# A three-stage fp32 chain on one core: two of four k-times-v products one step later, and a reordered change of stages

## The chip, the cores and the metric

The kernel runs on 1 core of one Trainium2 chip. The time is that of the device for one execution, in microseconds (us): 924.01 as the median of 3 runs (923.23 to 927.03). The engines have these names in the profile: PE is TensorE's matmuls and PEld its weight loads, DVE is VectorE, ACT is ScalarE, POOL is GpSimd, SP is the engine that issues the transfers (its queue reads SPq).

## The reference

```
kv  = einsum('bhsd,bhse->bhde', k, v)          # B=4, H=8, S=576, D=64
out = einsum('bhsd,bhde->bhse', q, kv)
rms = sqrt(mean(out * out, axis=-1) + 1e-6)
x   = out / rms * g_norm                       # then heads side by side: x is [2304, 512]
g   = x @ w_gate;  silu = g / (1 + exp(-g))    # w_gate, w_val: [512, 1536]
y   = (silu * (x @ w_val)) @ w_out             # w_out: [1536, 512]
h   = y @ w_in2                                # [512, 2048]
z   = (max(h, 0) + log1p(exp(-|h|))) @ w_out2  # [2048, 512]; the output, fp32
```

## The kernel before

There are three stages. The attention of batch 0 comes first (the first 35 us). Stage 1 is the gated layer: 6 chunks of 384 tokens (`NCH`) by 12 slices of 128 hidden columns (`NF1`), 72 steps k = 0..71, each with a chunk c and a slice f. The attention of batches 1 to 3 is laid between the steps of stage 1. Stage 2 is the second layer: 6 chunks by 16 slices (`NF2`).

Every matmul of the two layers is done in three passes on numbers split into a high part (rounded to the matmul's own format, fp32r) and a low part (the rest): lines L543, L544, L545. So each weight slice and each chunk of x has to be split first. For a weight slice, SP loads the raw numbers into one of two buffers (`stage1` or `stage2`), ACT copies them to the high part (L674 for stage 1, `split_high2` L681 for stage 2), and POOL subtracts that from the raw ones for the low part (L428, which counts `w_ready`). Only then may SP load the next slice but one into that buffer. The last slice of stage 2, f = 15, has both parts from POOL (L433 and L428). The slices of stage 2 take the places in `arena` that those of stage 1 leave: slice f may be written once the `down1` of a given step has been done (`slot_free2`).

A step k of stage 1 on PE is: gate(k), 12 matmuls into bank 0; val(k), 12 matmuls into bank 1; and down1(k-1), 12 matmuls that multiply the product of the step before by w_out. ACT makes silu of the gate (L695), DVE the gated product (`glu`: L881, then the split into g_hi at L872 and g_lo at L874). down1(k) waits for g_lo of step k (`g_split`).

Attention of batch b = 1, 2, 3: k times v of four pairs of heads (`pair`, L466, 20 small matmuls each). Pair 0 stands behind the gate of step `KV_AT[b]` (4, 17, 30), pair 1 behind its val, and pairs 2 and 3 both behind the gate of the next step. Pairs 0 and 2 share one buffer for k and v, pairs 1 and 3 another, so SP can issue the loads of pair 2 only when the product of pair 0 is done, and so for 3 and 1 (`next_pair`). DVE then copies the four products from PSUM into `kv_blocks` (`fill_blocks`, L773), two steps behind `KV_AT[b]` PE multiplies the first tile of q by it (`q_times_kv`, L481), and four more tiles follow, every second step. q comes turned by DVE (`turn_q`, L789).

SP works through one list in order. Around the attention of batch 1 that list is: weight slices 5, 6 and 7 of stage 1, then pairs 2 and 3 of batch 1, then slices 8 to 11.

At the change of stages (k = 71), before:

- PE: gate(71), val(71), down1(70), then up2(0,0) (stage 2, chunk 0, slice 0), then down1(71), then up2(0,1), up2(0,2), and from there up2 and down2 in turn. up2(0,0) needs the split x of chunk 0 (`xs_ready`), tile by tile, four tiles.
- DVE: the glu of step 70, then the split of x for stage 2 (`split_x`, L848 and L850 for each of four tiles), then the glu of step 71, then the softplus pieces of stage 2 (L892 to L899 and its own g_hi, g_lo). Tile t of the split may overwrite x_hi and x_lo once val(71) has read that tile (`xs_used`, `val_done`).
- ACT: silu(70), the high parts of slices 13 and 14, silu(71), the table of functions for stage 2, the four functions of the first softplus (L715 to L721), and then `store_y` (L705, four copies), which takes the sums of stage 1's last chunk out of PSUM.
- POOL: the low parts of slices 12, 13 and 14, and both parts of slice 15.

Of the kernel before, what the change touches and what calls it, by code (L numbers as in the profile page):

```python
# [45 lines left out]
BLK = 32  # L46
CB, BB = CH // BLK, S // BLK
POOL_HIGH = 1
ACT_HIGH2 = NF2 - 1
NATT = B - 1  # L50


# [25 lines left out]
def program(nc, ctx, q, k, v, g_norm, w_gate, w_val, w_out, w_in2, w_out2, out):  # L78
# [101 lines left out]
    def sem(name):  # L180
        return ctx.enter_context(nc.semaphore(name))
# [29 lines left out]
    w_hi_ready = sem("w_hi_ready")  # L211
    w_hi_ready_pool = sem("w_hi_ready_pool")
    w_ready = sem("w_ready")


    xs_hi_ready = sem("xs_hi_ready")
# [72 lines left out]
    def _(sp):  # L289
# [51 lines left out]
            sp.dma_start(stage1[:, s, 2 * KT * P:RAW1], w_out[f * P:(f + 1) * P, :]).then_inc(raw_loaded[s], 16)  # L341

        def load_step2(f):
            sp.wait_ge(w_ready, NF1 + f - 1)
            if f == 0:

                sp.wait_ge(kv_done, B * KT)
                sp.wait_ge(xn_ready, B * NT)
            s = f % 2
            sp.dma_start(stage2[:, s, 0:KT * P].rearrange("p (t n) -> p t n", t=KT),  # L350
                         w_in2[:, f * P:(f + 1) * P].rearrange("(t p) n -> p t n", p=P)).then_inc(raw_loaded[s], 16)
            sp.dma_start(stage2[:, s, KT * P:RAW2], w_out2[f * P:(f + 1) * P, :]).then_inc(raw_loaded[s], 16)
# [25 lines left out]
        load_q_blocks(1, 3)  # L378
        load_step1(5)
        load_step1(6)  # L380
        load_step1(7)
        next_pair(1, 2)
        next_pair(1, 3)
        for f in range(8, NF1):
            load_step1(f)
        for b in range(1, B):
            for j in range(3):
# [28 lines left out]
    @block.gpsimd  # L416
    def _(pool):
        nc.gpsimd.memset(eps[:, :], EPS).then_inc(zeros_ready, 1)
        nc.gpsimd.memset(kv_blocks[:, :, :], 0.0).then_inc(zeros_ready, 1)
        nc.gpsimd.memset(ident[:, :], 0.0).then_inc(zeros_ready, 1)  # L420
        pool.wait_ge(zeros_ready, 3)
        nc.gpsimd.affine_select(out=ident[:, :], in_=ident[:, :], compare_op=ALU.not_equal, fill=1.0, base=0,
                                pattern=[[-1, P]], channel_multiplier=1).then_inc(const_ready, 1)

        def split_rest(high, count, slot, raw, size):

            pool.wait_ge(high, count)
            nc.gpsimd.tensor_tensor(slot[:, size:2 * size], raw, slot[:, 0:size].bitcast(F32),  # L428
                                    ALU.subtract).then_inc(w_ready, 1)

        def split(n, count, slot, raw, size):
            pool.wait_ge(raw_loaded[n % 2], raw_count(n))
            nc.gpsimd.tensor_copy(slot[:, 0:size], raw).then_inc(w_hi_ready_pool, 1)  # L433
            split_rest(w_hi_ready_pool, count, slot, raw, size)

        for f in range(NF1):
            slot, raw = arena[:, f * SLOT1:(f + 1) * SLOT1], stage1[:, f % 2, :]
            if f < POOL_HIGH:  # L440
                split(f, f + 1, slot, raw, RAW1)
            else:
                split_rest(w_hi_ready, f - POOL_HIGH + 1, slot, raw, RAW1)
        for f in range(NF2):
            pool.wait_ge(down_done, slot_free2(f))
            slot, raw = arena[:, f * SLOT2:(f + 1) * SLOT2], stage2[:, f % 2, :]
            if f < ACT_HIGH2:
                split_rest(w_hi_ready, NF1 - POOL_HIGH + f + 1, slot, raw, RAW2)
            else:
                split(NF1 + f, POOL_HIGH + f - ACT_HIGH2 + 1, slot, raw, RAW2)  # L450


    @block.tensor
    def _(pe):
# [63 lines left out]
        def attention_after_gate(k):  # L518

            if k == 1:  # L520
                pe.wait_ge(x_ready, NT)
            for b in range(1, B):
                if k == KV_AT[b]:
                    pair(b, 0)
                if k == KV_AT[b] + 1:
                    pair(b, 2)
                    pair(b, 3)

# [60 lines left out]
        def up2(c, f):  # L589


            pe.wait_ge(w_ready, NF1 + f + 1)
            for t in range(KT):
                if f == 0:
                    pe.wait_ge(xs_ready, c * KT + (NCH * KT + t + 1))
# [26 lines left out]
        for k in range(1, STEPS1):  # L622
            up1(k)
            down1(k - 1)
        pe.wait_ge(silu_ready, STEPS1)
        up2(0, 0)
        down1(STEPS1 - 1)
        for f in range(1, LAG2):
            up2(0, f)
        with pe.Fori(0, NCH - 1) as c:  # L630
            for f in range(LAG2, NF2):
# [14 lines left out]
    def _(act):  # L646
# [92 lines left out]
        for k in range(1, STEPS1):  # L739
# [6 lines left out]
                root(b * NT, j)  # L746
            if k + 2 < NF1:
                split_high(k + 2)
            for f in range(ACT_HIGH2):
                if STEPS1 - NF1 + under(f) + 1 == k:  # L750
                    split_high2(f)
        nc.scalar.preload_act_table_set("natural_log_exp_and_others")
        softplus_terms(0, 0)
        store_y(NCH - 1)
        softplus_terms(0, 1)
        with act.Fori(0, NCH - 1) as c:
            for f in range(2, NF2):
# [10 lines left out]
    def _(dve):  # L768
# [107 lines left out]
        def glu(k):  # L876
# [6 lines left out]
            dve.wait_ge(g_ready, k + 1)  # L883
            split_g(k, 0, act_a[:, f % 2, :], g_hi[:, f % 2, :], g_lo[:, f % 2, :])

        def softplus(c, f):


# [16 lines left out]
        for k in range(STEPS1):  # L905
            c, f = divmod(k, NF1)
            for b in range(1, B):
                if k == KV_AT[b] + 1:
                    fill_blocks(b * KT, kv_ps)
            if k in TILE_OF:  # L910
                turn_q(*TILE_OF[k])
# [1 line left out]
                dve.wait_ge(x_ready, X_NEEDED[c + 1])  # L913
                split_x(c + 1, bass.ds(c * CB + CB, CB), val_done, k + 1)
            elif f == NF1 - 1:
                dve.wait_ge(acc_free, 2)
                split_x(NCH, bass.ds(0, CB), val_done, STEPS1, scaled=False)
            glu(k)
            if k in TILE_OF:
                b, j = TILE_OF[k]  # L920
# [1 line left out]
                normalize_turned(b, j)  # L922
            if k - TURN_AFTER in TILE_OF:
                turn_x(*TILE_OF[k - TURN_AFTER])
        with dve.Fori(0, NCH - 1) as c:
            for f in range(NF2 - 1):
                softplus(c, f)
# [27 lines left out]
```

## Time and profile before

| | |
|---|---|
| time, median of 3 runs | 924.01 us (923.23 to 927.03) |
| the profiled execution | 926.35 us, of which the span is 924.3 us and 2.05 us lie around it |
| PE busy in the span | 902.5 us (98%), 5128 matmuls |
| DVE busy | 526.9 us (57%) |
| ACT busy | 346.9 us (38%) |
| POOL busy | 84.6 us (9%) |
| mean granted clock of TensorE | 0.994 of full speed |
| chain that ended last | PE 91%, SPq 3%, DMA 2%, DVE 2%, POOL 1%, ACT 1% |

The busy time counts an instruction from its start to its end, and the matmuls overlap (one of 0.33 us starts every 0.17 us), so the start times on PE tell more than the busy share: where two rows of PE stand further apart than the matmuls between them take, PE stood still or ran slowly. The granted clock says at which share of 2.4 GHz TensorE ran in a stretch. The three stretches in which PE stands still for want of data, the start apart, lie at 64 to 70 us, at 161 us and at 511 to 519 us.

### The profile page before, as it was taken

How to read it: one execution, taken by the hardware profiler on the slowest of the kernel's cores; microseconds unless marked ns; L12 is line 12 of the kernel's file. 1: busy time of each engine (PE TensorE's matmuls, PEld its weight loads, DVE VectorE, ACT ScalarE, POOL GpSimd, SP SyncE). 2: the span in 40 equal slices, each digit the busy share in tenths (PEclk: the TensorE clock that was granted, in tenths of full speed). 3: DMA queues.
4: the chain of work that ended last, by engine and by line, in shares of the span. 5: the costliest groups of instructions: out<-in, count | busy, mean ns of one | idle time of the engine just before them, and what ended most of it. 6: DMA issues, size and time to landing. Idle time of an engine off the chain costs nothing.

```text
span 924.3 us, 13268 instructions
## 1 busy us (share of the span) xinstructions
PE 902.5 (98%) x5128; PEld 853.0 (92%) x5128; DVE 526.9 (57%) x1006; ACT 346.9 (38%) x602; POOL 84.6 (9%) x38
## 2 busy tenths in 40 slices
PE   6889999999999999999999899999999999999998
PEld 5779999999999999999999799998988998998997
DVE  3634652363245424214223887877878878878875
ACT  1433440243023301000233454545554544654543
POOL 2453300000000000000355200000000000000000
PEclk9999999999999999999999999999999999999999
DMA  9783362016211110000134000000000000000000
GB/s 222 171 198 92 93 137 64 23 35 143 59 23 46 39 42 1 1 1 1 45 116 137 23 1 1 34 0 0 34 0 0 34 0 0 34 0 0 35 1 35
DMA packets 84201, 44.38 MB, mean 48 GB/s; under 512 B 40768, under 2 KB 76736, under 8 KB 84160
## 3 DMA queue, kind: packets, MB, share of 16 engines
q1 hardware_dynamic: 84000, 43.80, 18.1%
q8 instruction: 30, 0.49, 0.2%
q14 instruction: 11, 0.09, 0.0%
q10 hardware_dynamic: 160, 0.00, 0.0%
HBM read 35.52 MB, written 8.26 MB: 47 GB/s over the span
## 4 chain that ended last, share of the span: by engine, by line
PE 91%; SPq 3%; DMA 2%; DVE 2%; POOL 1%; ACT 1%; issue 0%; DVEq 0%; ACTq 0%
PE bank L543 22%; PE bank L544 22%; PE bank L545 22%; PE bank L611 7%; PE bank L612 7%; PE bank L610 7%; PE bank L481 2%; SPq L316 1%; PE bank L466 1%; DMA v_rest<-in_v 1%; SPq L294 1%; POOL arena L428 1%; DVE x_lo L850 1%; SPq L339 1%; DMA v<-in_v 1%; DMA stage<-in_moe_w_out 0%
## 5 line engine op out<-in xcount | busy, mean ns | idle before, releaser
L543 PE MATMUL bank<-x_hi,arena 128*128 128x384 f32 x960 | 324.2, 338 | 5.6 <-DVE x_lo L850 3.5
L545 PE MATMUL bank<-x_hi,arena 128*128 128x384 f32 x960 | 322.7, 336 | 0.0
L544 PE MATMUL bank<-x_lo,arena 128*128 128x384 f32 x960 | 322.1, 336 | 0.0
L543 PEld LDWEIGHTS bank<-x_hi,arena 128*128 128x128 f32 x960 | 180.8, 188 | 12.5 <-DVE x_lo L850 3.7
L544 PEld LDWEIGHTS bank<-x_lo,arena 128*128 128x128 f32 x960 | 180.9, 188 | 3.8
L545 PEld LDWEIGHTS bank<-x_hi,arena 128*128 128x128 f32 x960 | 180.7, 188 | 0.0
L881 DVE TENSOR_TENSOR act_a<-act_a,bank 128x384 f32<-128x384 f32 x72 | 39.8, 553 | 231.5 <-PE bank L545 225.5
L695 ACT ACTIVATE act_a<-bank 128x384 f32<-128x384 f32 x72 | 35.3, 490 | 247.1 <-PE bank L545 246.8
L428 POOL TENSOR_TENSOR arena<-stage,arena 128x1024 fp32r<-128x1024 f32 (+1 forms) x28 | 80.8, 2895 | 414.0 <-ACT arena L681 370.1
L715 ACT ACTIVATE act_a<-bank 128x384 f32<-128x384 f32 x96 | 47.3, 493 | 189.1 <-PE bank L545 187.1
L612 PE MATMUL bank<-arena,g_lo 128*128 128x512 f32 x288 | 113.8, 395 | 0.0
L611 PE MATMUL bank<-arena,g_hi 128*128 128x512 f32 x288 | 113.6, 394 | 0.0
L610 PE MATMUL bank<-arena,g_hi 128*128 128x512 f32 x288 | 111.9, 389 | 0.0
L874 DVE TENSOR_TENSOR g_lo<-act_a,g_hi 128x384 fp32r<-128x384 f32 x168 | 100.2, 596 | 5.8
L543 PE MATMUL bank<-g_hi,arena 128*128 128x384 f32 x288 | 98.2, 341 | 0.0
L544 PE MATMUL bank<-g_lo,arena 128*128 128x384 f32 x288 | 96.4, 335 | 0.0
L545 PE MATMUL bank<-g_hi,arena 128*128 128x384 f32 x288 | 96.4, 335 | 0.0
L892 DVE SCALAR_TENSOR_TENSOR act_c<-act_w,act_u 128x384 f32<-128x384 f32 x96 | 53.4, 557 | 60.1 <-ACT act_w L719 60.1
L872 DVE CAST g_hi<-act_a 128x384 fp32r<-128x384 f32 x168 | 71.6, 426 | 7.6
L612 PEld LDWEIGHTS bank<-arena,g_lo 128*128 128x128 f32 x288 | 54.0, 187 | 11.5
L611 PEld LDWEIGHTS bank<-arena,g_hi 128*128 128x128 f32 x288 | 54.0, 188 | 9.3
L610 PEld LDWEIGHTS bank<-arena,g_hi 128*128 128x128 f32 x288 | 54.1, 188 | 8.8
(55 smaller groups left out, 795.6 us busy)
## 6 DMA issues: line engine op xcount, KB each, us to landing
stage<-in_moe_w_out SPq DMA_DIRECT2D x28, 256.0 KB, 3.4
out_dram<-out_stage SPq DMA_DIRECT2D x18, 256.0 KB, 2.1
k<-in_k SPq DMA_DIRECT2D x16, 256.0 KB, 3.2
v<-in_v SPq DMA_DIRECT2D x16, 256.0 KB, 3.3
stage<-in_moe_w_in SPq DMA_DIRECT2D x16, 256.0 KB, 2.6
xy<-in_q SPq DMA_DIRECT2D x48, 72.0 KB, 3.0
stage<-in_moe_w_gate SPq DMA_DIRECT2D x12, 256.0 KB, 3.3
stage<-in_moe_w_val SPq DMA_DIRECT2D x12, 256.0 KB, 3.5
```

The source lines that it names most:

```text
L428: nc.gpsimd.tensor_tensor(slot[:, size:2 * size], raw, slot[:, 0:size].bitcast(F32), ALU.subtract).then_inc(w_ready, 1)
L543: nc.tensor.matmul(ps, hi, rhs_hi, start=first, stop=False)
L544: nc.tensor.matmul(ps, hi, rhs_lo, start=False, stop=False)
L545: return nc.tensor.matmul(ps, lo, rhs_hi, start=False, stop=last)
L610: nc.tensor.matmul(acc_ps[t][:, :], g[0], w[0], start=(f == 0), stop=False)
L611: nc.tensor.matmul(acc_ps[t][:, :], g[0], w[1], start=False, stop=False)
L612: last = nc.tensor.matmul(acc_ps[t][:, :], g[1], w[0], start=False, stop=(f == NF2 - 1))
L715: nc.scalar.activation(a, hid_ps[f % RING2][:, 0:CH], ACT.Abs).then_inc(abs_ready, 1)
L872: nc.vector.tensor_copy(hi, g).then_inc(g_hi_ready, 1)
L874: nc.vector.tensor_tensor(lo, g, hi.bitcast(F32), ALU.subtract).then_inc(g_split, 1)
L881: nc.vector.tensor_tensor(act_a[:, f % 2, :], act_a[:, f % 2, :], val_ps[:, 0:CH], ALU.mult).then_inc(g_ready, 1)
L892: nc.vector.scalar_tensor_tensor(act_c[:, :], w, 1.0, u, ALU.subtract, ALU.subtract).then_inc(rest_ready, 1)
```

## The change

Attention: the products of pairs 2 and 3, and DVE's `fill_blocks` behind them, move from step `KV_AT[b] + 1` to `KV_AT[b] + 2` (steps 6, 19 and 32), the step in which the first q tile is multiplied. In SP's list the loads of pairs 2 and 3 of batch 1 come ahead of weight slice 7 and no longer behind it.

Change of stages: on PE down1(71) comes ahead of up2(0,0). On DVE the glu of step 71 comes ahead of the split of x. The low parts of slices 13, 14 and 15 are made by DVE (`split_late`, with a count of its own, `w_late_ready`) and no longer by POOL: 13 and 14 ahead of the glu of step 71, 15 behind the split of x. The high part of slice 15 is made by ACT as the others are, and `store_y` comes ahead of the first softplus.

DVE, the end of step 4 to the beginning of step 6 (act_a<-act_a,bank is the gated product, kv_blocks the copy of `fill_blocks`, q_t the turned q). Before:

```order
L881 TENSOR_TENSOR act_a<-act_a,bank 128x384
L872 CAST g_hi<-act_a 128x384
L874 TENSOR_TENSOR g_lo<-act_a,g_hi 128x384
L773 COPY kv_blocks<-bank 64x4x64 x2
L881 TENSOR_TENSOR act_a<-act_a,bank 128x384
L872 CAST g_hi<-act_a 128x384
L874 TENSOR_TENSOR g_lo<-act_a,g_hi 128x384
L789 STREAM_TRANSPOSE q_t<-xy 128x4x4x32
```

After:

```order
L884 TENSOR_TENSOR act_a<-act_a,bank 128x384
L875 CAST g_hi<-act_a 128x384
L877 TENSOR_TENSOR g_lo<-act_a,g_hi 128x384
L884 TENSOR_TENSOR act_a<-act_a,bank 128x384
L875 CAST g_hi<-act_a 128x384
L877 TENSOR_TENSOR g_lo<-act_a,g_hi 128x384
L776 COPY kv_blocks<-bank 64x4x64 x2
L792 STREAM_TRANSPOSE q_t<-xy 128x4x4x32
```

The copies to `kv_blocks` have moved behind the glu of step 5, right ahead of the first turn of q.

DVE at the change of stages, from the end of the glu of step 70 on (x_hi and x_lo are the split of x, arena<-stage_118,arena is a low part of a weight slice). Before:

```order
L874 TENSOR_TENSOR g_lo<-act_a,g_hi 128x384
L848 CAST x_hi<-xy 128x384
L850 TENSOR_TENSOR x_lo<-xy,x_hi 128x384
L848 CAST x_hi<-xy 128x384
L850 TENSOR_TENSOR x_lo<-xy,x_hi 128x384
L848 CAST x_hi<-xy 128x384
L850 TENSOR_TENSOR x_lo<-xy,x_hi 128x384
L848 CAST x_hi<-xy 128x384
L850 TENSOR_TENSOR x_lo<-xy,x_hi 128x384
L881 TENSOR_TENSOR act_a<-act_a,bank 128x384
L872 CAST g_hi<-act_a 128x384
L874 TENSOR_TENSOR g_lo<-act_a,g_hi 128x384
```

After:

```order
L877 TENSOR_TENSOR g_lo<-act_a,g_hi 128x384
L893 TENSOR_TENSOR arena<-stage_118,arena 128x1024 x2
L884 TENSOR_TENSOR act_a<-act_a,bank 128x384
L875 CAST g_hi<-act_a 128x384
L877 TENSOR_TENSOR g_lo<-act_a,g_hi 128x384
L851 CAST x_hi<-xy 128x384
L853 TENSOR_TENSOR x_lo<-xy,x_hi 128x384
```

Two low parts and the glu now stand ahead of the split of x, whose other three tiles follow, and behind them the third low part.

ACT at the same place, from the high parts of slices 13 and 14 on (act_a<-bank is first silu(71), then the first function of the softplus; xy<-bank is `store_y`). Before:

```order
L681 ACTIVATE arena<-stage_118 128x1024 x2
L695 ACTIVATE act_a<-bank 128x384
L752 ACT_TABLE_LOAD
L715 ACTIVATE act_a_0_97<-bank 128x384
L717 ACTIVATE act_u_0_98<-act_a_0_97 128x384
L719 ACTIVATE act_w_0_105<-act_u_0_98 128x384
L721 ACTIVATE act_a_0_97<-act_w_0_105 128x384
L705 ACTIVATE xy<-bank 128x12x32 x4
```

After:

```order
L684 ACTIVATE arena<-stage_118 128x1024 x2
L698 ACTIVATE act_a<-bank 128x384
L684 ACTIVATE arena<-stage_118 128x1024
L755 ACT_TABLE_LOAD
L708 ACTIVATE xy<-bank 128x12x32 x4
L718 ACTIVATE act_a_0_97<-bank 128x384
L720 ACTIVATE act_u_0_98<-act_a_0_97 128x384
L722 ACTIVATE act_w_0_105<-act_u_0_98 128x384
```

The high part of slice 15 and the four copies of `store_y` now stand ahead of the first softplus.

```diff
--- before.py
+++ after.py
@@ -46,7 +46,8 @@
 BLK = 32
 CB, BB = CH // BLK, S // BLK
 POOL_HIGH = 1
-ACT_HIGH2 = NF2 - 1
+
+LATE2 = NF2 - 3
 NATT = B - 1
 
 
@@ -211,6 +212,7 @@
     w_hi_ready = sem("w_hi_ready")
     w_hi_ready_pool = sem("w_hi_ready_pool")
     w_ready = sem("w_ready")
+    w_late_ready = sem("w_late_ready")
 
 
     xs_hi_ready = sem("xs_hi_ready")
@@ -341,7 +343,10 @@
             sp.dma_start(stage1[:, s, 2 * KT * P:RAW1], w_out[f * P:(f + 1) * P, :]).then_inc(raw_loaded[s], 16)
 
         def load_step2(f):
-            sp.wait_ge(w_ready, NF1 + f - 1)
+            if f - 2 >= LATE2:
+                sp.wait_ge(w_late_ready, f - 1 - LATE2)
+            else:
+                sp.wait_ge(w_ready, NF1 + f - 1)
             if f == 0:
 
                 sp.wait_ge(kv_done, B * KT)
@@ -378,10 +383,9 @@
         load_q_blocks(1, 3)
         load_step1(5)
         load_step1(6)
-        load_step1(7)
         next_pair(1, 2)
         next_pair(1, 3)
-        for f in range(8, NF1):
+        for f in range(7, NF1):
             load_step1(f)
         for b in range(1, B):
             for j in range(3):
@@ -441,13 +445,10 @@
                 split(f, f + 1, slot, raw, RAW1)
             else:
                 split_rest(w_hi_ready, f - POOL_HIGH + 1, slot, raw, RAW1)
-        for f in range(NF2):
+        for f in range(LATE2):
             pool.wait_ge(down_done, slot_free2(f))
             slot, raw = arena[:, f * SLOT2:(f + 1) * SLOT2], stage2[:, f % 2, :]
-            if f < ACT_HIGH2:
-                split_rest(w_hi_ready, NF1 - POOL_HIGH + f + 1, slot, raw, RAW2)
-            else:
-                split(NF1 + f, POOL_HIGH + f - ACT_HIGH2 + 1, slot, raw, RAW2)
+            split_rest(w_hi_ready, NF1 - POOL_HIGH + f + 1, slot, raw, RAW2)
 
 
     @block.tensor
@@ -522,7 +523,7 @@
             for b in range(1, B):
                 if k == KV_AT[b]:
                     pair(b, 0)
-                if k == KV_AT[b] + 1:
+                if k == KV_AT[b] + 2:
                     pair(b, 2)
                     pair(b, 3)
 
@@ -589,7 +590,10 @@
         def up2(c, f):
 
 
-            pe.wait_ge(w_ready, NF1 + f + 1)
+            if f >= LATE2:
+                pe.wait_ge(w_late_ready, f + 1 - LATE2)
+            else:
+                pe.wait_ge(w_ready, NF1 + f + 1)
             for t in range(KT):
                 if f == 0:
                     pe.wait_ge(xs_ready, c * KT + (NCH * KT + t + 1))
@@ -622,10 +626,9 @@
         for k in range(1, STEPS1):
             up1(k)
             down1(k - 1)
+        down1(STEPS1 - 1)
         pe.wait_ge(silu_ready, STEPS1)
-        up2(0, 0)
-        down1(STEPS1 - 1)
-        for f in range(1, LAG2):
+        for f in range(LAG2):
             up2(0, f)
         with pe.Fori(0, NCH - 1) as c:
             for f in range(LAG2, NF2):
@@ -746,12 +749,12 @@
                 root(b * NT, j)
             if k + 2 < NF1:
                 split_high(k + 2)
-            for f in range(ACT_HIGH2):
+            for f in range(NF2):
                 if STEPS1 - NF1 + under(f) + 1 == k:
                     split_high2(f)
         nc.scalar.preload_act_table_set("natural_log_exp_and_others")
+        store_y(NCH - 1)
         softplus_terms(0, 0)
-        store_y(NCH - 1)
         softplus_terms(0, 1)
         with act.Fori(0, NCH - 1) as c:
             for f in range(2, NF2):
@@ -883,6 +886,13 @@
             dve.wait_ge(g_ready, k + 1)
             split_g(k, 0, act_a[:, f % 2, :], g_hi[:, f % 2, :], g_lo[:, f % 2, :])
 
+        def split_late(f):
+
+            slot = arena[:, f * SLOT2:(f + 1) * SLOT2]
+            dve.wait_ge(w_hi_ready, NF1 - POOL_HIGH + f + 1)
+            nc.vector.tensor_tensor(slot[:, RAW2:SLOT2], stage2[:, f % 2, :], slot[:, 0:RAW2].bitcast(F32),
+                                    ALU.subtract).then_inc(w_late_ready, 1)
+
         def softplus(c, f):
 
 
@@ -905,7 +915,7 @@
         for k in range(STEPS1):
             c, f = divmod(k, NF1)
             for b in range(1, B):
-                if k == KV_AT[b] + 1:
+                if k == KV_AT[b] + 2:
                     fill_blocks(b * KT, kv_ps)
             if k in TILE_OF:
                 turn_q(*TILE_OF[k])
@@ -913,8 +923,8 @@
                 dve.wait_ge(x_ready, X_NEEDED[c + 1])
                 split_x(c + 1, bass.ds(c * CB + CB, CB), val_done, k + 1)
             elif f == NF1 - 1:
-                dve.wait_ge(acc_free, 2)
-                split_x(NCH, bass.ds(0, CB), val_done, STEPS1, scaled=False)
+                split_late(LATE2)
+                split_late(LATE2 + 1)
             glu(k)
             if k in TILE_OF:
                 b, j = TILE_OF[k]
@@ -922,6 +932,9 @@
                 normalize_turned(b, j)
             if k - TURN_AFTER in TILE_OF:
                 turn_x(*TILE_OF[k - TURN_AFTER])
+        dve.wait_ge(acc_free, 2)
+        split_x(NCH, bass.ds(0, CB), val_done, STEPS1, scaled=False)
+        split_late(LATE2 + 2)
         with dve.Fori(0, NCH - 1) as c:
             for f in range(NF2 - 1):
                 softplus(c, f)
```

## Rows read from the trace of the kernel before

**Rows 1.** Waits of PE: engine line, waited for: us in total, times, longest
```profile
PE bank L466 <- DMA v_rest<-in_v: 11.2, 4, 6.7
```

**Rows 2.** Timeline of PE, 63 to 82 us: start, length, instruction, [idle before it, releaser]
```profile
63.73 0.34 PE L545 MATMUL bank<-x_hi,arena 128*128 128x384 f32 x1
67.25 1.12 PE L466 MATMUL bank<-v,k 128*64 128x64 f32 x16 [3.18 <-DMA v_rest<-in_v]
...
70.65 0.69 PE L543 MATMUL bank<-x_hi,arena 128*128 128x384 f32 x1
...
73.85 0.33 PE L543 MATMUL bank<-g_hi,arena 128*128 128x384 f32 x1
...
80.09 1.05 PE L481 MATMUL bank<-kv_blocks,q_t 128*128 128x128 f32 x8
```

**Rows 3.** Timeline of PE, 158 to 167 us
```profile
159.72 0.34 PE L545 MATMUL bank<-x_hi,arena 128*128 128x384 f32 x1
...
162.74 0.44 PE L543 MATMUL bank<-x_hi,arena 128*128 128x384 f32 x1
```

**Rows 4.** Timeline of PE, 249 to 256 us
```profile
250.77 0.34 PE L545 MATMUL bank<-x_hi,arena 128*128 128x384 f32 x1
...
252.79 0.44 PE L543 MATMUL bank<-x_hi,arena 128*128 128x384 f32 x1
```

**Rows 5.** Timeline of SP, 60 to 68 us
```profile
61.53 0.43 SPq L294 DMA_DIRECT2D k<-in_k  x1
...
65.85 0.61 SPq L297 DMA_DIRECT2D v_rest<-in_v  x1
```

**Rows 6.** Timeline of POOL, 66 to 71 us
```profile
67.09 3.43 POOL L428 TENSOR_TENSOR arena<-stage,arena 128x1536 fp32r<-128x1536 f32 x1 [3.52 <-ACT arena L674]
```

**Rows 7.** Timeline of DVE, 160 to 168 us
```profile
162.86 0.88 DVE L773 COPY kv_blocks<-bank 64x256 f32<-64x256 f32 x2 [6.39 <-PE bank L466]
...
166.66 0.70 DVE L789 STREAM_TRANSPOSE q_t<-xy 128x512 f32<-128x512 f32 x1
```

**Rows 8.** Timeline of PE, 507 to 523 us
```profile
511.31 0.34 PE L545 MATMUL bank<-g_hi,arena 128*128 128x384 f32 x1
...
516.69 0.69 PE L543 MATMUL bank<-x_hi,arena 128*128 128x384 f32 x1 [3.00 <-DVE x_lo L850]
...
521.63 0.33 PE L543 MATMUL bank<-x_hi,arena 128*128 128x384 f32 x1
```

**Rows 9.** Busy time by stretch (us, PE PEld DVE ACT POOL, PEclk, DMA share, GB/s)
```profile
516.00:520.00 4.00, 3.28 (x9) 2.73 (x10) 2.85 (x6) 0.95 (x2) 0.22 (x1) 0.57 0.02 4
```

**Rows 10.** Timeline of DVE, 503 to 525 us
```profile
503.43 0.55 DVE L881 TENSOR_TENSOR act_a<-act_a,bank 128x384 f32<-128x384 f32 x1 [3.65 <-PE bank L545]
...
504.41 0.56 DVE L874 TENSOR_TENSOR g_lo<-act_a,g_hi 128x384 fp32r<-128x384 f32 x1
...
509.31 2.66 DVE L850 TENSOR_TENSOR x_lo<-xy,x_hi 128x384 fp32r<-128x384 f32 x1
...
512.28 0.56 DVE L850 TENSOR_TENSOR x_lo<-xy,x_hi 128x384 fp32r<-128x384 f32 x1
...
523.54 0.56 DVE L874 TENSOR_TENSOR g_lo<-act_a,g_hi 128x384 fp32r<-128x384 f32 x1
```

**Rows 11.** Timeline of POOL, 500 to 517 us
```profile
501.24 2.43 POOL L428 TENSOR_TENSOR arena<-stage,arena 128x1024 fp32r<-128x1024 f32 x1 [2.27 <-ACT arena L681]
506.64 4.92 POOL L428 TENSOR_TENSOR arena<-stage,arena 128x1024 fp32r<-128x1024 f32 x2 [2.98 <-ACT arena L681]
...
513.82 2.41 POOL L428 TENSOR_TENSOR arena<-stage,arena 128x1024 fp32r<-128x1024 f32 x1
```

**Rows 12.** Timeline of ACT, 505 to 523 us
```profile
507.12 1.07 ACT L681 ACTIVATE arena<-stage 128x1024 fp32r<-128x1024 f32 x1 [0.62 <-DMA stage<-in_moe_w_out]
...
508.57 1.28 ACT L752 ACT_TABLE_LOAD   x1
519.02 0.49 ACT L715 ACTIVATE act_a<-bank 128x384 f32<-128x384 f32 x1 [9.16 <-PE bank L545]
```

## The prediction

> **What bounds the kernel now.** The page comes first: PE is busy for 98% of the span and the chain that ended last is 91% PE. So only what makes PE stand still, or run slowly, is worth time. The table of PE's waits names the transfer of k and v as the largest [rows 1]: 11.2 us in four waits, of which the longest, 6.7 us, belong to the loads at the very start, which the change leaves alone. The timeline of PE then shows where it loses time, and I measure that between starts, since a matmul's length overlaps the next. Undisturbed, 36 matmuls take 80.09 - 73.85 = 6.24 us, so one takes 0.1733 us [rows 2].
>
> Three places stand out. At 64 us PE waits for k and v of pairs 2 and 3 of batch 1 [rows 2], at 161 us for those of batch 2 [rows 3], at 511 us for the split x of stage 2 [rows 8]. Batch 3 passes the same place with no wait [rows 4]. Behind a stand of 3.00 us [rows 8] the granted clock is low: from 516 to 520 us it is 0.57 on the mean, so mostly the lower level of 1.2 GHz [rows 9].
>
> **Batch 1.** The gate of step 5 ends at 63.73 + 0.17 = 63.90, and down1(4) begins at 73.85 [rows 2]. Between them lie two products (40 small matmuls) and val(5): 9.95 us. Undisturbed, the two products cost 252.79 - 250.94 = 1.85 us (batch 3, [rows 4]), val 12 x 0.1733 = 2.08, and the first matmul behind them starts its successor about 0.1 late (0.44 long in place of 0.33). That is 4.03. The loss is 5.9 us: the waits, and val at the lower clock (from 70.65 to 73.85 its 12 matmuls took 3.20 and not 2.08).
>
> After the change PE runs val(5), down1(4) and gate(6), 36 matmuls, before it wants pairs 2 and 3: at 63.90 + 6.24 = 70.14, with its usual gap at 70.4. In the trace both pairs had landed about a microsecond before PE went on at 70.65 [rows 2], although their eight issues, from 61.53 to 65.85 + 0.61 = 66.46 [rows 5], stood behind the three of weight slice 7. SP now issues them ahead of those, so they land 1.5 us earlier at least. The wait goes whole: gain 5.9, lower bound 5.
>
> What the move pushes back is slice 7. At worst its three issues end where the pairs' ended, 66.46 in place of 61.5, 5 us later. Its low part was ready at 67.09 + 3.43 = 70.52 [rows 6], so then at 75.5. up1(7) begins after the products (1.95), val(6), the q tile (0.8) and down1(5), at about 77.1. Slice 7 is hidden, by 1.6 us in the worst case.
>
> DVE's copies to kv_blocks (0.88) now stand straight ahead of the turn of q (0.70) [rows 7], and both must be through before the first q tile. They start 0.12 behind the products and last 1.58, so they end 1.70 behind; PE has val in between, 2.08 and 0.1. Margin 0.5 us, at steps 6, 19 and 32. Behind the waiting copies DVE has the turn and the glu of the same step, which needs val anyway. Cost 0; from below nothing can be gained there, from above it is the margin overrun, taken up as a rival.
>
> **Batch 2.** 162.74 - 159.89 = 2.85 us for two products [rows 3] against 1.85. SP's issues stay where they are and PE comes a step, 6.24 us, later. Gain 1.0. **Batch 3** had no wait: 0.
>
> **Change of stages.** down1(70) ends at 511.48, up2(0,1) begins at 521.63 [rows 8]. Between them lie the 24 matmuls of up2(0,0) and down1(71), 4.16 us undisturbed; it took 10.15. The loss is 5.99, the most this part can give. I follow DVE to see what stays.
>
> Two x_lo of the same shape take 0.56 and 2.66 us [rows 10]; the long one ran from 509.31 to 511.97, while POOL was in its low parts, 506.64 to 511.56, and a second one as long beside POOL's of 513.82 [rows 11]. After the change POOL's last work is slice 12, over at 501.24 + 2.43 = 503.67. So DVE works at its short times. The Trainium skill (SBUF — State Buffer, "SBUF: two separate sides") says why: VectorE and GpSimd share one port pair as an exclusive lock, taken by a VectorE operation with two SBUF inputs against a GpSimd one that reads SBUF. By that rule moving three low parts from POOL to DVE takes the blocking away for the whole change of stages; were it a slowness of DVE's own there, the sum would be that of the second rival. The rows agree with the rule so far.
>
> A low part on DVE (1024 elements) is in no row. Bounds: 0.56 (384 elements, [rows 10]) and POOL's 2.43 [rows 11]. ACT's copies of these sizes stand as 1.07 to 0.49 [rows 12]; 0.56 x 1.07 / 0.49 = 1.22, in proportion to the elements it would be 1.49. I take 1.22. The Trainium skill (VectorE: DVE Perf Modes, "The TRN2 errata") gives (N + 151) / 0.96 ns for such a subtraction, an estimate of 1.22 as well; no row here shows it.
>
> Slice 13 can start when POOL started it, 506.64, slice 14 when ACT's copy ends, 507.12 + 1.07 = 508.19 [rows 11, 12]. DVE is through with both at 508.25 + 1.22 = 509.5. The glu of step 71 follows that of step 70 by 6.24: 503.43 + 6.24 = 509.67 [rows 10], when val(71) is done. So they fit, by 0.2. g_lo ends 504.97 - 503.43 = 1.54 later, at 511.21, and PE wants it at 511.48: no stall, margin 0.27.
>
> Then the split of x: cast and subtraction are at most 1.54 - 0.55 = 0.99 a tile, so the tiles are ready at 512.2, 513.2, 514.2, 515.2. PE, with down1(71) ahead, wants them at 513.56, 514.08, 514.60, 515.12. Only the last is close, 0 to 0.1 us.
>
> Next in line is the first softplus. SP may load slice 15 when DVE has slice 13 done, 507.9; before, it was at 509.1, and POOL had cast it and gone on at 513.82, about 3.6 us after issue plus a cast of 1.1. So it lands at 511.5. ACT may write its place when down1(70) is done, 511.65; copy 1.07, table 1.28, four copies of `store_y` at most 0.49 each [rows 12]: ACT is free at 516.0 at the latest. up2(0,0) ends at 515.64, so ACT costs 0.1. From the first function to g_lo took 524.10 - 519.02 = 5.08 [rows 10, 12]: 521.1. PE wants it after three more up2, at 515.64 + 6.24 = 521.88. Margin 0.8. The third low part fits in DVE's wait before it. Where the stall goes, nothing else is late.
>
> **Sum.** 5.9 + 1.0 + 6.0 = 12.9; 0.2 off for the two tight handovers: 12.7. Span 924.3 - 12.7 = 911.6, with the 2.05 around it 913.65 for the profiled execution. That execution (926.35) was 2.3 above the median of the runs, 924.01, so against the median the forecast is **911.3**.
>
> **Rivals.**
> (A) A low part on DVE takes its upper bound, 2.43. Then both are done at 506.64 + 4.86 = 511.5, g_lo at 513.0, PE stands 1.5 us, the tiles of x follow at PE's pace. 912.8. For it: no row of the operation. Against: ACT's ratio.
> (B) The long x_lo is not POOL's doing. Then the split begins at 511.2 and goes as slowly as before: the third tile came 516.69 - 509.31 = 7.4 us after the first x_lo began, so at about 519, wanted at 514.6; 4.4 lost and 1 more at the lower clock. 916.7. Against: 0.56 at 512.28, in POOL's pause between 511.56 and its cast.
> (C) The 5.9 of batch 1 is given back at the weights: PE reaches up1(7) to up1(11) 6 us earlier, and the two raw buffers, ACT and POOL may not keep up. 917.2. Against: in ACT's order slice 8 and later stand behind the functions of PE's own q tiles, so they move with PE; slice 7 is hidden by 1.6.
> (D) Slower. At steps 6, 19 and 32 PE waits for kv_blocks and the turned q, with down1 queued behind. It decides from 0.5 us of lateness on DVE, one to one, three times. To eat 12.7 us DVE must be 4.7 late at each; at 5.5 late it is 15 lost, 926.3. Against: DVE is idle for 6.39 us ahead of its copies [rows 7], and POOL, which could stretch DVE, works only near the first of the three.
> (E) The change does not do what it says, both waits stay: 924.
>
> **How the numbers follow.** Forecast 0.77, A 0.10, B 0.04, C 0.06, D 0.01, E 0.02. A change under 0.5% (4.6 us) could not be told from none. Faster: forecast, A, B, C and some of D's small cases, 0.97; same 0.02; slower 0.01. The range, 909.7 to 916.0, takes the whole 12.9, 1.4 for the spread of such medians (the runs before lie 923.23 to 927.03), and A with as much above it, most of what B and C lose.
>
> **What the profile after would show.** Right: no wait for k and v but at the start; two products in step 6, at about 70.4 us; val at 0.1733 a matmul; the L853 subtractions at 0.56 throughout; a low part on DVE of about 1.2 us, two of them over by 502.6 (509.5 less 6.9); no PEclk below 1.00 after the start. Wrong: PE rows with a wait for `w_ready` in steps 7 to 11, for kv_blocks or q_t in steps 6, 19, 32, for g_lo at the change, or x_lo still over 2 us with POOL at rest.

## The result, and the profile after

The changed kernel takes 913.30 us in the median of 4 runs (912.77 to 915.10), the kernel before 925.26 in 4 runs beside it (923.23 to 927.03). The ratio is 0.9869, 95% interval 0.9848 to 0.989: 1.3% faster. The profiled execution took 912.80 us with a span of 911.0 and a mean granted clock of 1.00 (before: 926.35, 924.3 and 0.994).

The page of the changed kernel, PE's row of part 1 and the chain that ended last:

```profile
PE 896.5 (98%) x5128; PEld 849.2 (93%) x5128; DVE 524.8 (58%) x1009; ACT 348.1 (38%) x603; POOL 76.0 (8%) x34
...
PE 97%; DVE 1%; SPq 1%; DMA 1%; ACT 0%; issue 0%; ACTq 0%
```

PE's busy time is 6.0 us less: 2.3 of it lie in the stretch of batch 1 and 2.5 at the change of stages, where matmuls ran at the lower clock or were drawn out by a wait, and 0.8 lie in the first 38 us, which the change leaves alone. The chain is now 97% PE. PE's two longest waits in the span (answers to [rows 1]):

```profile
PE bank L467 <- DMA v_rest<-in_v: 6.9, 1, 6.9
PE bank L544 <- DVE x_lo L848: 1.9, 3, 0.9
```

The 11.2 us in four waits for v_rest have become one of 6.9, the loads at the very start. L848 is the split of x for stage 1, in the first steps; L853, that for stage 2, is no longer among them.

Step 6 of the changed kernel on PE (answers to [rows 2]): the last matmul of gate(6), the two products, val(6), the first q tile.

```profile
69.57 0.34 PE L546 MATMUL bank<-x_hi,arena 128*128 128x384 f32 x1
69.84 0.69 PE L467 MATMUL bank<-v,k 128*64 128x64 f32 x16
...
70.71 0.69 PE L467 MATMUL bank<-v,k 128*64 128x64 f32 x16
...
71.59 0.44 PE L544 MATMUL bank<-x_hi,arena 128*128 128x384 f32 x1
...
73.78 0.94 PE L482 MATMUL bank<-kv_blocks,q_t 128*128 128x128 f32 x7
```

From 69.57 + 0.17 to 71.59 are 1.85 us, the undisturbed price of [rows 4]. DVE beside it (answers to [rows 7]):

```profile
71.71 0.88 DVE L776 COPY kv_blocks<-bank 64x256 f32<-64x256 f32 x2 [4.32 <-PE bank L467]
72.62 0.71 DVE L792 STREAM_TRANSPOSE q_t<-xy 128x512 f32<-128x512 f32 x1
74.48 0.55 DVE L884 TENSOR_TENSOR act_a<-act_a,bank 128x384 f32<-128x384 f32 x1 [1.15 <-PE bank L546]
```

The copies start 0.12 behind the products and the turned q is ready at 73.33; PE wants it at 73.78. Margin 0.45.

The change of stages, PE: last matmul of down1(70), first of down1(71), last of it, first of up2(0,0) and of up2(0,1) (answers to [rows 8]).

```profile
503.98 0.33 PE L546 MATMUL bank<-g_hi,arena 128*128 128x384 f32 x1
504.15 0.33 PE L544 MATMUL bank<-g_hi,arena 128*128 128x384 f32 x1
...
506.06 0.33 PE L546 MATMUL bank<-g_hi,arena 128*128 128x384 f32 x1
506.23 0.33 PE L544 MATMUL bank<-x_hi,arena 128*128 128x384 f32 x1
...
508.31 0.33 PE L544 MATMUL bank<-x_hi,arena 128*128 128x384 f32 x1
```

24 matmuls in 508.31 - 504.15 = 4.16 us; it was 10.15. DVE there (answers to [rows 10]):

```profile
499.20 1.23 DVE L893 TENSOR_TENSOR arena<-stage,arena 128x1024 fp32r<-128x1024 f32 x1 [1.56 <-ACT arena L684]
500.97 1.22 DVE L893 TENSOR_TENSOR arena<-stage,arena 128x1024 fp32r<-128x1024 f32 x1 [0.55 <-ACT arena L684]
502.34 0.55 DVE L884 TENSOR_TENSOR act_a<-act_a,bank 128x384 f32<-128x384 f32 x1
...
503.32 0.56 DVE L877 TENSOR_TENSOR g_lo<-act_a,g_hi 128x384 fp32r<-128x384 f32 x1
...
506.78 0.56 DVE L853 TENSOR_TENSOR x_lo<-xy,x_hi 128x384 fp32r<-128x384 f32 x1
...
513.04 0.56 DVE L877 TENSOR_TENSOR g_lo<-act_a,g_hi 128x384 fp32r<-128x384 f32 x1
```

A low part on DVE (L893) takes 1.23 and 1.22 us. g_lo is ready at 503.88 for a PE that wants it at 504.15, every x_lo takes 0.56, and the last is ready at 507.34, when PE wants it at 507.79. ACT there (answers to [rows 12]):

```profile
504.35 1.06 ACT L684 ACTIVATE arena<-stage 128x1024 fp32r<-128x1024 f32 x1 [3.03 <-PE bank L546]
505.43 1.28 ACT L755 ACT_TABLE_LOAD   x1
506.72 1.64 ACT L708 ACTIVATE xy<-bank 128x384 f32<-128x384 f32 x4
508.51 0.49 ACT L718 ACTIVATE act_a<-bank 128x384 f32<-128x384 f32 x1
```

ACT is through with `store_y` at 508.36 and begins the first softplus at 508.51, when up2(0,0) is done; g_lo of slice 0 is ready at 513.60 and down2(0,0) begins at 514.55.

**Where the 13.3 us of the span came from.** Same place in both traces, the kernel before less the changed one: 38.52 - 38.46 = 0.06 at down1(0); 80.09 - 73.78 = 6.31 at the first q tile of batch 1; 7.33 at the gated product of step 70 (503.43 [rows 10]; in the changed kernel that of step 71 at 502.34, less the 6.24 of a step, 496.10); 521.63 - 508.31 = 13.32 at up2(0,1); 920.68 - 907.36 = 13.32 at the last matmul. So 6.25 at batch 1, 1.0 at batch 2, 6.0 at the change of stages, nothing anywhere else. The medians are 12.0 us apart and not 13.3: the profiled execution of the kernel before lies 1.1 us above its median of 925.26, that of the changed kernel 0.5 below its own.

### The profile page after: what moved, and what is told of

Its sections match the earlier page's. It is cut to its first block, busy times and chain, and to the rows that moved or that the text cites. A ratio compares the mean times of both kernels' runs of the same rounds, so it can differ in the third digit from the quotient of the medians.

```text
span 911.0 us, 13266 instructions
## 1 busy us (share of the span) xinstructions
PE 896.5 (98%) x5128; PEld 849.2 (93%) x5128; DVE 524.8 (58%) x1009; ACT 348.1 (38%) x603; POOL 76.0 (8%) x34
## 4 chain that ended last, share of the span: by engine, by line
PE 97%; DVE 1%; SPq 1%; DMA 1%; ACT 0%; issue 0%; ACTq 0%
PE bank L544 24%; PE bank L545 24%; PE bank L546 24%; PE bank L615 7%; PE bank L616 7%; PE bank L614 7%; PE bank L482 2%; PE bank L467 1%; DMA v<-in_v 1%; SPq L296 0%; DVE sums L820 0%; DVE x_norm L829 0%; DVE x_lo L848 0%; DVE x_hi L846 0%; SPq L364 0%; DVE q_t L783 0%
## 5 line engine op out<-in xcount | busy, mean ns | idle before, releaser
L432 POOL TENSOR_TENSOR arena<-stage,arena 128x1024 fp32r<-128x1024 f32 (+1 forms) x25 | 73.4, 2946 | 403.2 <-ACT arena L684 366.0
L877 DVE TENSOR_TENSOR g_lo<-act_a,g_hi 128x384 fp32r<-128x384 f32 x168 | 97.0, 578 | 5.8
L875 DVE CAST g_hi<-act_a 128x384 fp32r<-128x384 f32 x168 | 74.7, 444 | 7.6
```

Source lines behind the costliest of these rows:

```text
L875: nc.vector.tensor_copy(hi, g).then_inc(g_hi_ready, 1)
L877: nc.vector.tensor_tensor(lo, g, hi.bitcast(F32), ALU.subtract).then_inc(g_split, 1)
```

## The experiments

The loads at the very start land at another time in each execution: the first product begins at 6.7 to 8.1 us and down1(0) at 38.5 to 41.0, and with them moves the whole span. From down1(0) to the last matmul the profiled executions agree to some hundredths where nothing differs, so the comparisons below take that length ("the length" from here on):

| kernel | down1(0) to last matmul | median of runs | ratio to before, 95% |
|---|---|---|---|
| before | 882.16 | | |
| changed | 868.90 | 913.30 | 0.9869 (0.9848 to 0.989) |
| 1 attention part alone | 875.89 | 920.46 | 0.9932 (0.9911 to 0.9953) |
| 2 change of stages alone | 874.39 | 919.08 | 0.9924 (0.9901 to 0.9946) |
| 3 slice 7 ahead of the pairs | 868.93 | 913.41 | 0.9869 (0.9842 to 0.9896) |
| 4 low parts on DVE, old order | 869.98 | 914.96 | 0.9873 (0.9852 to 0.9894) |
| 5 low parts on POOL, new order | 871.91 | 917.37 | 0.9905 (0.9883 to 0.9927) |
| 6 low parts behind the glu | 872.04 | 916.63 | 0.9903 (0.9875 to 0.9931) |
| 7 `store_y` behind the softplus | 868.89 | 913.64 | 0.9874 (0.9845 to 0.9903) |
| 8 memsets on POOL | 869.76 | 914.47 | 0.9883 (0.9856 to 0.991) |

The ratios are to runs of the kernel before in the same sitting (medians 925.26, 927.14 and 925.70).

**1. The attention part alone.** The kernel before with (the change of the step stands in PE's list and in DVE's)

```diff
-                if k == KV_AT[b] + 1:
+                if k == KV_AT[b] + 2:
-        load_step1(7)
         next_pair(1, 2)
         next_pair(1, 3)
-        for f in range(8, NF1):
+        for f in range(7, NF1):
```

> The attention part alone (products of pairs 2 and 3 and kv_blocks a step later, their loads ahead of weight slice 7), the change of stages as before. Theory, the two parts are independent: PE gains 5.9 us at batch 1 and 1.0 at batch 2 and nothing is given back at the change of stages, so the span is 924.3 - 6.9 = 917.4 (916.9 to 917.6), and the stretch of 10.15 us at the change of stages stands as it was, 7 us earlier. Rival, the stalls feed each other (POOL, ACT and the raw buffers reach the change of stages in another state): that stretch changes by more than 0.5 us. Second rival, the weights of slices 7 to 11 bind once PE comes earlier: part of the 5.9 comes back as waits for POOL's low parts.

Span 919.1, 1.5 more than the upper end of what was expected; 1.0 of that is the later start (down1(0) at 39.53 and not 38.52). In the length it gains 6.27 and not 6.9. From down1(0) to the first q tile it takes 74.85 - 39.53 = 35.32, as the changed kernel (73.78 - 38.46), so no weight binds. What is missing is at the change of stages. PE there (the last start before the long wait, the first behind it, and a matmul of down1(71)):

```profile
507.11 0.33 PE L544 MATMUL bank<-x_hi,arena 128*128 128x384 f32 x1
510.45 0.69 PE L542 MATMUL bank<-x_hi,arena 128*128 128x384 f32 x1 [3.01 <-DVE x_lo L849]
...
515.49 0.49 PE L544 MATMUL bank<-g_hi,arena 128*128 128x384 f32 x1
```

The wait is the same, 3.01 us, but the matmuls stay 0.32 apart from 510.45 until 515.8, 5.4 us; in the kernel before they did from 516.69 until 519.8, 3.1 us. The stretch took 11.1 us and not 10.15, which is more than the 0.5 us that the rival named. The granted clock shows where the rest comes from. One microsecond of PE's stand, first in the kernel before, then in experiment 1 (views of busy time by stretch, as [rows 9]):

```profile
515.00:516.00 1.00, 0.00 (x0) 0.00 (x0) 1.00 (x1) 0.00 (x0) 1.00 (x1) 1.00 0.00 0
509.00:510.00 1.00, 0.00 (x0) 0.00 (x0) 1.00 (x1) 0.00 (x0) 0.98 (x1) 0.50 0.00 0
```

In the kernel before the clock fell to 0.50 at 516.6, when PE went on, and rose at 520.0; in experiment 1 it had fallen at 509.0, while PE stood, and rose at 515.8. Half of the time in which matmuls ran at it, 1.6 or 2.7 us, is what it adds to the same wait. Whether the change or the execution moved the fall, one trace of each does not show. That the clock differs without any change is on record: its mean over the span was 0.990 to 0.996 in the 15 executions of the kernel before that ran beside these experiments.

**2. The change of stages alone.** The changed kernel with (again in both lists)

```diff
-                if k == KV_AT[b] + 2:
+                if k == KV_AT[b] + 1:
+        load_step1(7)
         next_pair(1, 2)
         next_pair(1, 3)
-        for f in range(7, NF1):
+        for f in range(8, NF1):
```

> The change of stages alone, the attention as before. Theory: 6.0 us off, span 918.3 (918.0 to 918.8), the waits for k and v of 3.2 and 0.9 us and the low granted clock at 64 to 75 us stand as before, no low clock at 516 us. Rival, the two parts are not independent: the sum of the two gains differs from the 13.3 us that both together give in the span by more than 0.5 us.

Span 917.3, 7.0 off and not 6.0, and 7.8 in the length. PE at batch 1: the last gate matmul and the two products.

```profile
64.12 0.34 PE L547 MATMUL bank<-x_hi,arena 128*128 128x384 f32 x1
66.53 0.69 PE L468 MATMUL bank<-v,k 128*64 128x64 f32 x16 [2.07 <-DMA v_rest<-in_v]
...
68.57 0.63 PE L468 MATMUL bank<-v,k 128*64 128x64 f32 x14 [1.10 <-DMA v_rest<-in_v]
```

Both k and v came about 1 us earlier in this execution, measured from the end of the gate, and the wait of 0.24 us at 53.32 in the kernel before (see below) is absent; so down1(0) to the q tile took 40.19 and not 41.57. Batch 2 waits 0.38 us in place of 0.93, and batch 3 loses 0.15 where it lost nothing. At the change of stages there is no wait and no low clock. Both parts together gain 13.26, the two alone 6.27 and 7.77, sum 14.04: 0.78 apart, so the gains differ by more than the 0.5 us of the rival. But this does not show that one part acts on the other. The 1.38 us less at batch 1 lie in a stretch in which this kernel gives every engine the same work as the kernel before; they are a difference between two executions.

**3. SP's list.** The changed kernel with slice 7 ahead of the pairs.

```diff
+        load_step1(7)
         next_pair(1, 2)
         next_pair(1, 3)
-        for f in range(7, NF1):
+        for f in range(8, NF1):
```

> The changed kernel with SP's list as before: weight slice 7 of stage 1 ahead of the loads of pairs 2 and 3 of batch 1. The loads at the very start land at another time in every execution, so the time is taken from down1(0) to the last matmul: 868.9 us in the changed kernel. Theory, the later step alone does it: both pairs land some 0.3 to 1 us before PE wants them in step 6, so 868.9 to 869.4. Rival, the moved loads carry the gain: PE waits a microsecond or more for v in step 6, 870 or more.

868.93 against 868.90, no wait in step 6. SP starts to issue the last of the eight loads at 65.45 (61.39 in the changed kernel), the products start at 71.25, undisturbed (this execution runs 1.4 us late from the start):

```profile
71.25 0.69 PE L468 MATMUL bank<-v,k 128*64 128x64 f32 x16
...
72.12 0.69 PE L468 MATMUL bank<-v,k 128*64 128x64 f32 x16
...
75.19 1.05 PE L483 MATMUL bank<-kv_blocks,q_t 128*128 128x128 f32 x8
```

So the later step does it, and the place in SP's list is worth nothing on top of it.

**4. and 5. Who makes the low parts, and in which order.** Two kernels, and with experiment 1 and the changed kernel all four combinations. In 4 the low parts stay on DVE and the old order returns:

```diff
                 split_late(LATE2)
                 split_late(LATE2 + 1)
+                dve.wait_ge(acc_free, 2)
+                split_x(NCH, bass.ds(0, CB), val_done, STEPS1, scaled=False)
             glu(k)
...
+        up2(0, 0)
         down1(STEPS1 - 1)
-        for f in range(LAG2):
+        for f in range(1, LAG2):
```

> The changed kernel with the old order on PE and DVE: the split of x ahead of the glu of step 71, up2(0,0) ahead of down1(71); the three low parts stay on DVE. Theory, the long x_lo is POOL's doing, and the order is worth little: the split runs at 0.87 us a tile from 502.2 to 505.7, the glu follows to 507.2, PE waits some 1.0 us for g_lo, span 912.0 (911.8 to 912.4). Rival, the long x_lo is DVE's own there (as in the kernel before): x_lo of 2 us and more again, PE waits 4 us or more, span 915 or more.

Its span is 914.6, outside both, because the start came 2.5 us late (down1(0) at 40.95) and nothing else: in the length it is 1.08 over the changed kernel, where the theory had 1.0. DVE's operations are all short, and PE waits once, for g_lo (ready at 509.63):

```profile
508.69 0.34 PE L546 MATMUL bank<-x_hi,arena 128*128 128x384 f32 x1
509.68 0.44 PE L544 MATMUL bank<-g_hi,arena 128*128 128x384 f32 x1 [0.66 <-DVE g_lo L878]
```

In 5 the order is the new one and POOL makes the low parts of slices 13 to 15:

```diff
-LATE2 = NF2 - 3
+LATE2 = NF2
...
-                split_late(LATE2)
-                split_late(LATE2 + 1)
...
-        split_late(LATE2 + 2)
```

> The changed kernel with the three low parts back on POOL (the high part of slice 15 stays with ACT); PE and DVE keep the new order. Theory of the shared port: the cast to g_hi at the change of stages waits for the end of POOL's second low part (about 1.4 us long in place of 0.36), g_lo is ready about 1.3 us late, PE waits about 1.1 us; the split of x is then free until POOL starts slice 15, so at most one x_lo is 2 us or longer: span 912 to 914.5. Rival, the order alone brings the gain and POOL does not matter: span 911.0 to 911.3, all DVE operations at their short times. Second rival, DVE is as slow as before in all of the split: span 915 or more.

871.91, 3.01 over the changed kernel. Its span, 915.5, lies above the theory's 912 to 914.5, of which 1.45 us are the later start (down1(0) at 39.91). DVE and POOL of that kernel:

```profile
504.37 1.41 DVE L875 CAST g_hi<-act_a 128x384 fp32r<-128x384 f32 x1
...
506.68 0.56 DVE L853 TENSOR_TENSOR x_lo<-xy,x_hi 128x384 fp32r<-128x384 f32 x1
...
508.02 2.58 DVE L851 CAST x_hi<-xy 128x384 fp32r<-128x384 f32 x1
```

```profile
500.75 4.82 POOL L432 TENSOR_TENSOR arena<-stage,arena 128x1024 fp32r<-128x1024 f32 x2 [2.94 <-ACT arena L684]
507.94 2.44 POOL L432 TENSOR_TENSOR arena<-stage,arena 128x1024 fp32r<-128x1024 f32 x1 [2.37 <-ACT arena L684]
```

The cast at 504.37 is 1.41 long and ends just behind POOL's second low part (505.57); that of 508.02 is 2.58 long and ends just behind slice 15 (510.38). The others are short. Two long operations, both over with POOL's. PE waits 0.67 us for g_lo and then 1.42 for an x_lo, which came late because the cast ahead of it was the long one; the theory had 1.1 for g_lo and one long x_lo at most. The granted clock stays at 1.00 here and in experiment 4.

So, from the attention part alone (875.89): new order alone 3.98 us, low parts on DVE alone 5.91, both 6.99. Experiment 1 also has slice 15 wholly on POOL and `store_y` behind the softplus, and 1 us more of low clock than the kernel before; against a stall at the price of the kernel before each of the three figures would be about 1 us less (an estimate: 11.1 less 10.15).

**6. The low parts behind the glu.**

```diff
-                split_late(LATE2)
-                split_late(LATE2 + 1)
             glu(k)
...
+        split_late(LATE2)
+        split_late(LATE2 + 1)
         dve.wait_ge(acc_free, 2)
         split_x(NCH, bass.ds(0, CB), val_done, STEPS1, scaled=False)
```

> The changed kernel with the low parts of slices 13 and 14 behind the glu of step 71 on DVE in place of ahead of it. Theory, two chains with little margin: the first tile of x is ready 2.45 us later, 1.0 later than PE wants it, and at 0.87 us a tile against PE's 0.52 the loss grows to 2.0 at the fourth tile; the load of slice 15 leaves SP 4.7 us later, ACT makes its high part, the table and store_y behind it, and the first softplus begins 4 us late against a margin of 1.5 and the 2.0 that PE is late anyway: PE waits 0.5 to 1.5 us more, for g_lo ahead of down2(0,0). Together 2.5 to 3.5 us, 871.4 to 872.4 from down1(0) to the last matmul. Rival, only the split of x counts: 870.9, no wait for g_lo. Second rival, the place does not matter as DVE has 43% of idle time: 868.9 to 869.3.

872.04, 3.14 over. PE waits for the first tile of x, then a little for each of the other three, and for g_lo ahead of down2(0,0):

```profile
508.55 0.41 PE L544 MATMUL bank<-x_hi,arena 128*128 128x384 f32 x1 [0.77 <-DVE x_lo L853]
...
509.32 0.44 PE L544 MATMUL bank<-x_hi,arena 128*128 128x384 f32 x1
...
518.97 0.49 PE L614 MATMUL bank<-arena,g_hi 128*128 128x512 f32 x1 [0.88 <-DVE g_lo L877]
```

ACT shows why the last one: it stands 7.01 us for the raw slice 15, and `store_y` and the first softplus (from 513.72) follow behind.

```profile
509.84 1.06 ACT L684 ACTIVATE arena<-stage 128x1024 fp32r<-128x1024 f32 x1 [7.01 <-DMA stage<-in_moe_w_out]
510.92 1.28 ACT L755 ACT_TABLE_LOAD   x1
```

Both chains that the prediction found narrow are narrow.

**7. `store_y`.** The changed kernel with

```diff
-        store_y(NCH - 1)
         softplus_terms(0, 0)
+        store_y(NCH - 1)
```

> The changed kernel with store_y behind the first softplus on ACT, as in the kernel before. Theory, ACT has time: the first softplus can't begin before up2(0,0) is done, so g_lo of slice 0 comes as it does; that of slice 1 some 0.4 us later, wanted by PE 2 us after; no wait, 868.9 (868.8 to 869.1) from down1(0) to the last matmul. Rival, this move carries part of the gain, since stage 2 begins 6 us earlier against ACT's work: PE waits at one of the first down2, 869.5 or more.

868.89. The move is worth nothing; g_lo of slice 1 comes 0.25 later against g_lo of slice 0 and nobody waits.

**8. Which DVE operations POOL blocks.** The changed kernel with this on POOL behind its last low part (and ACT waits for the last memset ahead of the loop of stage 2):

```diff
+        pool.wait_ge(val_done, STEPS1)
+        for n in range(6):
+            nc.gpsimd.memset(squares[:, :], 0.0).then_inc(zeroed, 1)
+            pool.wait_ge(zeroed, n + 1)
```

> The changed kernel with work added on POOL alone: six memsets of 128x512, which read nothing from SBUF, one behind the other from the moment when val(71) is done, so beside DVE's glu and the split of x (ACT waits for their end once, before the loop of stage 2). Theory of one exclusive port pair, as the low parts showed it for POOL operations that read SBUF: DVE's casts with one SBUF input (0.36 us) stretch to the end of a memset, and its subtractions with two SBUF inputs (0.56) do so only if a POOL operation that merely writes blocks them too. If both are blocked, the split takes 2 us and more longer and PE waits 1 to 3 us; if only the casts are, some casts are 0.5 to 1 us, all x_lo 0.56 to 0.6, and PE waits under 1.5 us. Rival, POOL work of any kind beside DVE costs nothing and the long operations came from somewhere else: all at their short times, 868.9.

869.76, 0.86 over. DVE and POOL:

```profile
502.99 0.55 DVE L890 TENSOR_TENSOR act_a<-act_a,bank 128x384 f32<-128x384 f32 x1 [0.20 <-PE bank L551]
503.57 0.69 DVE L881 CAST g_hi<-act_a 128x384 fp32r<-128x384 f32 x1
504.29 0.56 DVE L883 TENSOR_TENSOR g_lo<-act_a,g_hi 128x384 fp32r<-128x384 f32 x1
504.77 0.75 DVE L857 CAST x_hi<-xy 128x384 fp32r<-128x384 f32 x1
505.55 0.56 DVE L859 TENSOR_TENSOR x_lo<-xy,x_hi 128x384 fp32r<-128x384 f32 x1
...
507.29 0.35 DVE L857 CAST x_hi<-xy 128x384 fp32r<-128x384 f32 x1
```

```profile
502.94 3.63 POOL L455 MEMSET squares<- 128x512 f32 x6 [5.96 <-PE bank L551]
```

While the memsets run (502.94 to 506.57) three casts take 0.69, 0.75 and 0.75 us in place of 0.36; the subtractions with two SBUF inputs stay at 0.56, and the product that reads PSUM at 0.55. Behind the memsets a cast takes 0.35 again. The three casts are 1.11 us longer together; the last tile of x is late by so much, and PE picks up the 0.86 in short gaps of 0.1 to 0.2 us ahead of down1(71) and of the tiles of x. A POOL operation that only writes draws out the casts and not the subtractions; the low parts, which read SBUF, drew out both (2.66 on x_lo in [rows 10], 1.41 on the cast of experiment 5).

## Why the prediction was right

The forecast was 911.3 within 909.7 to 916.0, the measured median 913.3. Its expected ratio, 911.3 / 924.0 = 0.9863, lies in the interval 0.9848 to 0.989. The span was forecast at 911.6 and is 911.0. The mechanism came as forecast at all three places; the weak step is the one from the span to the median. It took off 2.3 us, by which the profiled execution of the kernel before lay above its median, and that did not recur: the profiled execution of the changed kernel lies 0.5 below its median. So the median is 2.0 above the forecast though the span is 0.6 below.

- Batch 1, 5.9: 6.25 measured from down1(0) to the q tile. The 0.35 more is luck: in the kernel before PE stood 0.24 us ahead of its start at 53.32, with a slower first matmul behind it, until POOL had the low part of slice 4 ready (53.26). That lies ahead of all that the change touches, and neither the changed kernel nor experiments 1 and 2 have it. The products cost 1.85 and began at 69.84. The prediction puts the loss down to the waits and to val at the lower clock; the products ran at it too (1.12 in [rows 2], 0.69 in the changed kernel; the clock at 0.50 from 66.0), but it measured the whole stretch, so the sum has them.
- SP's moved loads ("Slice 7 is hidden, by 1.6 us in the worst case."): its low part was ready at 73.54 and PE began up1(7) at 76.76, 3.2 later. Experiment 3 gives 0.03 us for the move, experiment 1 no wait for weights. Rival C is out.
- kv_blocks and q_t, margin 0.5: 0.45, and no wait at any of the three steps. Rival D is out.
- Batch 2, 1.0: 1.0 in this pair of traces. In experiment 2, where the transfer came sooner, the same stall cost 0.45.
- Change of stages, 5.99 less 0.2 for tight handovers: 5.99; the 0.2 did not occur. The low part at 1.22 was 1.23 and 1.22, so rival A is out. By the estimate from the Trainium skill (VectorE: DVE Perf Modes, "The TRN2 errata"), whose formula is stated for an fp32 add of two tensors, it was 1.22; the trace agrees.
- The long x_lo as POOL's doing: experiment 5 brings the long operations back with POOL's work, two of them, and 4 shows the old order without them. Rival B is out. What the prediction did not read is that in the kernel before two casts of the split were long as well:

```profile
508.11 1.18 DVE L848 CAST x_hi<-xy 128x384 fp32r<-128x384 f32 x1 [3.14 <-PE bank L545]
...
512.76 1.19 DVE L848 CAST x_hi<-xy 128x384 fp32r<-128x384 f32 x1
```

The first ended 0.2 us behind POOL's first low part there (506.64 + 2.43 = 509.07), the other, at 513.95, 0.2 behind POOL's own cast of slice 15 (512.60 to 513.73). The two casts and the two x_lo are together some 5.9 us longer than the short ones. The Trainium skill (SBUF — State Buffer, "SBUF: two separate sides") says that VectorE's two-port modes meet any GpSimd operation in the lock on the shared port pair, and operations with two SBUF inputs only one that reads SBUF. The trace of experiment 8 agrees: casts 0.69 and 0.75 for 0.36, subtractions 0.56.

- ACT's chain with a margin of 0.8 to down2(0,0): 0.95 (513.60 to 514.55). Experiment 6 overran it, and PE waited.
- The split of x, last tile 0 to 0.1 us late: it was 0.45 early, since a tile takes 0.87 and not the 0.99 taken as its upper bound.

What the prediction treated as fixed and is not: the price of a stall. The 10.15 us at the change of stages were 11.1 in experiment 1, and the 41.57 from down1(0) to the q tile were 40.19 in experiment 2. That the terms came out to some tenths therefore owes something to the pair of executions that was profiled. And the spans differ at the very start by up to 2.5 us, more than the term of batch 2 and the 0.2 for the handovers together.

## What to carry to other kernels

When the bounding engine waits for another one, read how long each of the other's operations takes there against the same shape elsewhere: two x_lo of 2.66 and 2.65 us among those of 0.56 told that the work to move was POOL's. Moving it gave 5.9 of 7.0 us where a better order alone gave 4.0 (the stall of experiment 1, at its price). Let a transfer be wanted one step later rather than issued sooner, if the consumer of its result has the room; here the later step gave all of the 5.9 us at batch 1 and the earlier issue 0.03. And compare traces between two instructions behind the start, not by the span, when the start alone differs by up to 2.5 us from one execution to the next.

## What the runs showed of the hardware

- A POOL memset that only writes SBUF draws a DVE cast (fp32 from SBUF to SBUF, 128x384) out from 0.36 to 0.75 us and leaves a subtraction with two SBUF inputs at 0.56 and a product with one input in PSUM at 0.55; a POOL subtraction that reads SBUF drew the cast and the subtraction out, to 2.58 and 2.66, and left the product at 0.55 (experiment 5, at 503.78).
- Behind the same wait of 3.0 us the matmuls started 0.32 us apart and not 0.17 for 3.1 us in one execution and for 5.4 in another, so the same stall cost 6.0 or 7.0 us. The clock fell to 1.2 GHz at the end of the stand in the one and 1.5 us earlier, within it, in the other. Behind waits of 2.07 and 1.10 us at 64 to 68 us (experiment 2) it fell too, at 69.4, and rose at 72.8.
